# Making the token operand sums of a two-layer gated MLP on VectorE instead of Pool

## The reference

```
attention, per batch b (8) and head h (8), S = 576 tokens, D = 64:
    kv  = k^T v                      # 64 x 64
    o   = q kv                       # no softmax
    x   = o / sqrt(mean(o*o) + 1e-6) * g_norm
x: 4608 tokens x 512
layer 1:  x = (sigmoid(x Wg) * (x Wv)) Wo        # 512 -> 1536 -> 512
layer 2:  g = x Wg2;  x = (g * sigmoid(g) * (x Wv2)) Wo2
```

## Time and profile before

| what | value |
|---|---|
| time, median of 3 runs | 1890.42 us (1886.0 to 1890.89) |
| the profiled execution's own time | 1887.9 us |
| its span | 1886.1 us |
| mean granted TensorE clock | 0.98 of 2.4 GHz |
| busy share, TensorE / VectorE / ScalarE / Pool | 94% / 69% / 47% / 25% |
| Pool's four sums, 12 each | 22.8 + 24.5 + 26.6 + 22.8 us |
| VectorE's split of a token operand, 60 + 24 | mean 1209 and 1055 ns |

### The profile page before, as it was taken

One profiled execution on the slowest core, in us unless ns is written; L12 is line 12 of the kernel. 1 busy time (PEld: TensorE's weight loads), 2 busy tenths in 40 slices (PEclk: granted clock), 3 DMA queues, 4 the chain that ended last, 5 costly groups with the idle time before them and its releaser, 6 DMA issues.

```text
span 1886.1 us, 30995 instructions
## 1 busy us (share of the span) xinstructions
PE 1774.4 (94%) x11184; PEld 1729.8 (92%) x11184; DVE 1297.9 (69%) x1993; ACT 892.7 (47%) x1676; POOL 462.8 (25%) x374
## 2 busy tenths in 40 slices
PE   6898999999999999999987999998999998999997
PEld 5787898899999999999987999998999998999997
DVE  3566767777765678666678777777767778766665
ACT  3555655555444445444354444444444444544444
POOL 5623323213211124111135011113211124111111
PEclk9999999999999999999999899999999999999998
DMA  8677587556655666665555544545665565555452
GB/s 204 211 220 235 185 252 237 190 183 202 229 187 208 209 223 226 210 212 185 185 179 190 185 161 174 185 167 197 214 208 186 184 220 195 172 182 182 183 183 75
DMA packets 201561, 368.52 MB, mean 195 GB/s; under 512 B 49856, under 2 KB 161472, under 8 KB 201408
## 3 DMA queue, kind: packets, MB, share of 16 engines
q1 hardware_dynamic: 201408, 366.53, 58.0%
HBM read 234.36 MB, written 130.55 MB: 193 GB/s over the span
## 4 chain that ended last, share of the span: by engine, by line
PE 71%; DVE 10%; issue 7%; DMA 4%; POOL 3%; SPq 2%; ACT 2%; POOLq 0%; DVEq 0%; ACTq 0%
PE ps L687 68%; DVE arena L1075 2%; DVE xo L984 2%; DVE hop L1036 2%; DVE arena L1088 1%; PE ps L595 1%; PE ps L628 1%; POOL rrms L1210 1%; DVE arena L1103 1%; DMA wops<-in_moe_w_gate_dram 1%; DMA x<-wops 1%; DMA wops<-in_v_dram 1%; DVE wa L979 1%; DMA wops<-in_q_dram 1%; PE ps L580 1%
## 5 line engine op out<-in xcount | busy, mean ns | idle before, releaser
L687 PE MATMUL ps<-xo,wa 128*128 128x384 f32 x6048 | 1087.0, 337 | 16.0 <-ACT arena L845 8.7
L687 PEld LDWEIGHTS ps<-xo,wa 128*128 128x128 f32 x6048 | 1051.1, 189 | 22.6 <-ACT arena L845 11.1
L687 PE MATMUL ps<-hop,wb 128*128 128x384 f32 x3024 | 562.7, 345 | 53.7 <-DVE arena L1088 23.4
L1075 DVE TENSOR_TENSOR arena<-ps,arena 128x384 f32<-128x384 f32 x648 | 351.2, 552 | 366.6 <-PE ps L687 287.0
L687 PEld LDWEIGHTS ps<-hop,wb 128*128 128x128 f32 x3024 | 541.6, 194 | 65.9 <-DVE arena L1088 25.3
L845 ACT ACTIVATE arena<-ps 128x384 f32<-128x384 f32 x648 | 317.4, 491 | 595.1 <-PE ps L687 583.2
L1292 POOL TENSOR_TENSOR arena<-arena 128x384 f32<-128x384 f32 x144 | 144.7, 1028 | 762.6 <-DVE arena L1075 762.6
L1036 DVE TENSOR_TENSOR hop<-arena,hop 128x384 fp32r<-128x384 f32 (+1 forms) x396 | 304.8, 792 | 37.2 <-ACT hop L827 31.2
L827 ACT ACTIVATE hop<-arena 128x384 fp32r<-128x384 f32 (+1 forms) x396 | 233.4, 608 | 66.7 <-DVE arena L1103 38.7
L866 ACT ACTIVATE arena<-arena 128x384 f32<-128x384 f32 x216 | 112.6, 521 | 118.2 <-DVE arena L1075 118.2
L1103 DVE TENSOR_TENSOR arena<-arena 128x384 f32<-128x384 f32 x216 | 143.3, 664 | 13.5
(11 more groups left out here) (61 smaller groups left out, 972.7 us busy)
## 6 DMA issues: line engine op xcount, KB each, us to landing
xo<-x_operands SPq DMA_DIRECT2D x168, 768.0 KB, 6.3
x_operands<-xo SPq DMA_DIRECT2D x84, 768.0 KB, 4.6
x<-arena SPq DMA_DIRECT2D x120, 384.0 KB, 3.3
arena<-x SPq DMA_DIRECT2D x96, 384.0 KB, 4.4
xraw<-x SPq DMA_DIRECT2D x22, 768.0 KB, 6.7
out_dram<-wops SPq DMA_DIRECT2D x48, 192.0 KB, 2.1
wops<-in_k_dram SPq DMA_DIRECT2D x22, 288.0 KB, 4.5
wops<-in_v_dram SPq DMA_DIRECT2D x22, 288.0 KB, 5.3
```

The source lines that it names most:

```text
L687: mm = pe.matmul(dst, lhsT, rhs, start=(pr in (1, 5, 2) and c == 0 and i == 0), stop=(c == 1 and i == 2), skip_group_check=(pr in (6, 7, 4 ...
L1075: nc.vector.tensor_tensor(dst, acc, buf, ALU.add).then_inc(summed, 1)
```

## The change

Pool no longer makes the token sums. VectorE makes all four with the same operands: `x_s1_s3` (s1 and, after it, s3), `x_s2` and `x_s4`. In a preparing stage s1 and s3 stand in window 2 where split 5 stood; after total(22,1) come split 5 and s2; split 6 stays. s4 and split 7 go to the head of window 0 of the next stage, ahead of splits 4 and 3. X_ORDER has 6 before 7. ScalarE's halves: split 5 at slot 7, split 6 at slot 9 as before, split 7 at slot 13. The DRAM store of operand 7 is issued in the next stage. For block 0 VectorE does s1, s3, split 5, s2, split 6 ahead of the loop, and s4, split 7 in stage 0.

```diff
-X_ORDER = (1, 2, 5, 7, 6, 4, 3)
+X_ORDER = (1, 2, 5, 6, 7, 4, 3)
...
-            for pr in X_ORDER[2:5]:
+            for pr in X_ORDER[2:4]:
                 store_xo(0, pr)
...
                 if first_pass(qq):
-                    for pr in X_ORDER[5:]:
+                    for pr in X_ORDER[4:]:
                         store_xo(qq, pr)
...
-                if prepares:
-                    store_xo(nxt, X_ORDER[4])
...
                             if is_late(u - 1):
                                 unit_xT(u - 1)
-                            if w == 2 and prepares:
-                                split_x(nxt, 5)
                         if s == 7:
                             copy(7, 0)
                             if w < 2:
...
                             if w == 2 and prepares:
-                                split_x(nxt, 7)
+                                split_x(nxt, 5)
...
                         if s == 12 and w == 2 and p == 0:
                             copy_c21(1)
-                        if s == 13 and is_late(u):
-                            unit_xT(u)
+                        if s == 13:
+                            if w == 2 and prepares:
+                                split_x(nxt, 7)
+                            if is_late(u):
+                                unit_xT(u)
...
+            a11, a12, a21, a22 = xraw[:, 0, 0:2], xraw[:, 0, 2:4], xraw[:, 1, 0:2], xraw[:, 1, 2:4]
+
+            def x_s1_s3(qq):
+                if qq == 0:
+                    for filled in x_filled:
+                        dve.wait_ge(filled, 48)
+                else:
+                    for loaded in xraw_loaded:
+                        dve.wait_ge(loaded, 16 * prep(qq))
+                nc.vector.tensor_tensor(xs, a21, a22, ALU.add).then_inc(xs_made, 1)
+                dve.wait_ge(xs_made, 4 * prep(qq) + 1)
+                nc.vector.tensor_tensor(a21, a11, a21, ALU.subtract).then_inc(xs_made, 1)
+
+            def x_s2(qq):
+                dve.wait_ge(x_lo, n_x(qq, 1))
+                dve.wait_ge(xs_made, 4 * prep(qq) + 2)
+                nc.vector.tensor_tensor(a11, xs, a11, ALU.subtract).then_inc(xs_made, 1)
+
+            def x_s4(qq):
+                dve.wait_ge(x_lo, n_x(qq, 5))
+                dve.wait_ge(xs_made, 4 * prep(qq) + 3)
+                nc.vector.tensor_tensor(xs, a12, a11, ALU.subtract).then_inc(xs_made, 1)
+
...
-            for pr in X_ORDER[2:5]:
-                split_x(0, pr)
+            x_s1_s3(0)
+            split_x(0, 5)
+            x_s2(0)
+            split_x(0, 6)
...
                         if w == 0 and first_pass(qq):
+                            x_s4(qq)
+                            split_x(qq, 7)
                             split_x(qq, 4)
                             split_x(qq, 3)
...
                         total(11, 0)
                         hop_split(3, None)
                         if prepares:
-                            split_x(nxt, 5)
+                            x_s1_s3(nxt)
                         total(22, 0)
                         if is_late(u):
                             unit_scale(u)
                         total(11, 1)
                         total(22, 1)
                         if prepares:
-                            split_x(nxt, 7)
+                            split_x(nxt, 5)
+                            x_s2(nxt)
...
-            x_s1(0)
-            x_s3(0)
-            x_s2(0)
-            x_s4(0)
...
-                if prepares:
-                    x_s1(nxt)
-                u = late_unit(qq, 2)
-                if is_late(u):
-                    rsqrt(u)
-                if prepares:
-                    x_s3(nxt)
-                    x_s2(nxt)
-                    x_s4(nxt)
-                if is_late(u + 1):
-                    rsqrt(u + 1)
+                for u in range(late_unit(qq, 2), late_unit(qq, 2) + 2):
+                    if is_late(u):
+                        rsqrt(u)
```

More of the change, by code:

```diff
@@ L1220, in differences @@
                 nc.gpsimd.tensor_tensor(st[:, 6], st[:, 3], st[:, 5], ALU.subtract).then_inc(t_made, 1)
[L1222 to L1245, removed]
             for t in range(STEPS):
@@ L1259, in _ @@
                 nxt = qq + 1
-                prepares = first_pass(nxt)
                 first_unit = 6 * (qq // NB + 1) if blk == NB - 1 and nxt < QN else None
```

## The result

| | before | after |
|---|---|---|
| time, median | 1890.66 us (1886.0 to 1891.87, 4 runs) | 1856.95 us (1854.75 to 1858.37, 4 runs) |
| the profiled execution, its span | 1887.9, 1886.1 us | 1854.75, 1853.0 us |

The account below looks back on a forecast made before the run. TensorE bounds the kernel, held by VectorE's chain that Pool's sums stretch by 4.3 us. Terms -18.5 - 1.4 - 2.9 - 3.1 - 7.3 = -33.2 gave 1854.7 us profiled, median 1857; range 1840 to 1876.

Parts of the forecast that it names:

- Rival 2: VectorE's chain before window 2: lengthening not from Pool, nothing gained there and tails paid, about 1915 us; chance 0.05.
- entry: Entry to window 2, stages 19 to 22: 0.55 us of waiting left of 4.20, and the clock stays up.
- tail: End of window 2, every prepared stage: waits of 0.7 before product 3 and 0.9 before the next stage, together 1.6 us.
- rival 1: Tail of window 2 is longer, 3.2 us, since ScalarE stands twice before a late VectorE sum: 1875 us; chance 0.15.
- rival 4: Tail of window 2 hides, bank waits only 0.3 us: 14 us better, 1843 us; chance 0.12.
- rival 3: Gain given back to the second-slowest chain, entry waits near 2.5 us, clock still falling: about 1871 to 1885; chance 0.11.
- The 1.68 us wait for hidden operand 7 stays: Stages 0 to 2: this wait remains because Pool's rsqrt starts in front of it; these stages -3.1 us in all.
- the store of operand 7: DMA queue at the next stage's head: it moves behind the next unit's loads, is read one pass later, costs nothing.
- stage 3: Wait of 2.88 us shrinks to 0.45, tail costs 1.4: -2.9 us.
- Stage 17: Pool's weight differences take the place of its sums in window 2, where the wait was 2.54 us: -0.8 in all.
- Stage 18: -3.0 us from additions L1292 no longer late, and -3.5 from the shrunken wait of 7.36 us.
- the term of -3.5: Stage 18: wait of 7.36 us shrinks to 2.8, with half of the clock's loss left standing.

Follow-up runs that it names:

- Experiment 1: The kernel before, with each of Pool's four token sums covering one column of 384 (results wrong): 1826.49 us, ratio 0.968.
- Experiment 3: The changed kernel's order of splits, stores and X_ORDER, with the four sums made by Pool at their places of before: 1901.81 us, ratio 1.0079.
- experiment 4: The changed kernel with three idle Pool instructions (96x768, two SBUF inputs) added in each of stages 17 to 22: 1882.01 us, ratio 0.9981.
- Experiment 6: The changed kernel, with the next attention unit's loads in window 2 issued ahead of the store of operand 5 in the DMA queue: 1852.4 us, ratio 0.9807.
- Experiment 10: The changed kernel with unit loads earlier in the DMA queue in windows 0, 1 and 2, copies ahead of split 6, s3 behind total(22,0): 1833.22 us.
- experiment 2: The changed kernel, with each of VectorE's four token sums covering one column of 384 (results wrong): 1838.76 us, ratio 0.9746.

## Why the prediction was right

*What bounds the kernel, and why.* This is right, and shown: experiments 1, 3 and 4 remove, keep and restore the wait with the reading Pool work alone. Rival 2 (the lengthening isn't Pool's) fell with the changed kernel's 0.55 us silu and with experiment 4. The rule of the Trainium skill, "SBUF — State Buffer", section "Who interferes with whom", says as well that a GpSimd instruction which only writes doesn't contend; the 0.55, 0.56 and 0.95 us beside eight memsets agree.

*Entry and tail.* The entry was predicted at 0.55 us, and 0.7 was found. The tail was predicted at 0.7 + 0.9 = 1.6. The rows show 0.48 and 0.50 of idle time (0.65 and 0.67 with the pipelined end), and taking both waits away brings the stage from 45.99 to 44.43 us, so it is 1.56. Rivals 1 (3.2 us) and 4 (0.3 us) are out, and rival 3 as well: no entry wait of 2.5 us is left.

*The rest of the sum is right partly by luck.* That the profiled execution came out at 1854.75 us, where 1854.7 was forecast, is chance: the parts outside stages 19 to 22 and stage 4 were off by up to 2.3 us each way and cancelled. These steps were wrong:

- "The 1.68 us wait for hidden operand 7 stays, because Pool's rsqrt starts in front of it": wrong in its cause. In the kernel before, the two splits of 5.08 us at 141.34 had two Pool instructions beside them:
```profile
140.60 2.96 POOL L1210 TENSOR_TENSOR rrms<-msq,mhalf 96x12 f32<-96x12 f32 x1 [7.50 <-DVE msq L999]
141.34 2.59 DVE L1036 TENSOR_TENSOR hop<-arena,hop 128x768 fp32r<-128x768 f32 x1
...
143.53 2.08 POOL L1235 TENSOR_TENSOR xraw<-xraw 128x768 f32<-128x768 f32 x1
```
  After, the rsqrt is still there and the splits are short:
```profile
142.31 2.94 POOL L1238 TENSOR_TENSOR rrms<-msq,mhalf 96x12 f32<-96x12 f32 x1 [8.74 <-DVE msq L998]
...
143.04 1.84 DVE L1061 TENSOR_TENSOR hop<-arena,hop 128x768 fp32r<-128x768 f32 x2
```
  In the whole kernel after, 15 splits of 128x768 ran beside an rsqrt and no other Pool instruction, and took 0.94 to 0.97 us each. In the kernel before three of them also touched s3's record, one in each of stages 0 to 2, and took 2.58. Experiment 1 shows the same pair at 1.84 us beside the rsqrt (2.94 us at 141.88), in the old order, with s3 of one column behind it. So the lengthening goes with s3's size and not with the rsqrt. How is open: the first split ends at 143.93, 0.4 us after s3's recorded start, so it was late before the record shows s3 at work (a Pool span in the records is rough). Window 2 of stage 0 fell from 26.12 to 22.39 us.
- The queue of DMAs. I priced the store of operand 7 at nothing and overlooked that of operand 5: it now waits for the later split 5 and holds the next attention unit's loads, issued at 151.62 where they were issued at 150.23, while TensorE wants v 1.4 us earlier (at 156.18, not 157.57). The wait that this leaves, in the timeline after:
```profile
151.22 0.35 SPq L408 DMA_DIRECT2D x_operands<-xo  x1
151.62 0.43 SPq L342 DMA_DIRECT2D wops<-in_k_dram  x1
...
158.07 0.92 PE L578 MATMUL ps<-wops 96*64 96x64 f32 x24 [1.89 <-DMA wops<-in_v_dram]
```
  There are two more like it, 1.99 (229.57) and 1.94 us (298.64), in stages 2 and 3, and none at these places before. A fourth, of 1.97 at 183.34, is not new: in the kernel before it is 2.57 (182.29). Experiment 6 shows that the three new ones come from the queue's order; with them gone stage 3 is 3.3 us shorter than before, where 2.9 was predicted and 0.6 measured. Experiment 10 gives 14 us more, but it goes further than undoing what the change did to the queue: it also takes away waits that the kernel before had.
- Stage 17. The wait of 2.54 us for a split of a hidden operand is gone, but the wait for a product behind the first step has grown from 1.36 to 2.95 us (972.10), and product 3 waits 1.32 us. Before, it was
```profile
977.45 7.58 PE L687 MATMUL ps<-hop,wb 128*128 128x384 f32 x42 [1.36 <-DVE arena L1103]
```
  Stage 17 is 1.0 us longer, not 0.8 shorter.
- Stage 18. It gained 9.35 us where 6.5 was predicted. The wait fell from 7.36 to 2.65, close to the 2.8 predicted, but the term of -3.5 does not follow from its own numbers: 7.36 - 2.8 is 4.6 already, half of the clock's loss is 1.3 more, and a tail of 1.6 goes the other way, together -4.3. Measured are -4.71 for this wait and +0.51 for window 2 behind it, thus -4.2. The other -5.15 lie in windows 0 and 1, where -3.0 was predicted for the additions L1292.
- The order of the work. The sum prices the later places of splits and stores at nothing except in the tail. Experiment 3 (15 us slower than before) and the pair of experiments 1 and 2 (12 us) show that it costs more, in stages 0 to 3 above all. Experiment 1 shows what the end of the contention is worth by itself in stages 0 to 3, 17.4 us; the change kept 5.9 of it, and the sum said 6.0. That is right, but with a gain and a cost that are both larger than the sum had them.

## What to carry to other kernels

A Pool instruction costs what VectorE can't do while it runs, not its own busy time: look for VectorE instructions with two SBUF inputs that take a multiple of their usual time beside one, while PSUM readers keep theirs, and move the work there if VectorE is the engine that the bottleneck waits for. When a stall goes, the next wait is often in the queues: read for each DMA queue which store is held by a later producer, and what loads stand behind it. Waits on one chain must be taken away together: here the first alone gave 0.1 us a stage, the last alone 0.8, and both 1.56.

## What the runs showed of the hardware that was not expected

A long Pool instruction need not hold VectorE: the 96x12 rsqrt ran for 2.94 us with two splits inside it that took their usual 1.84 together, though both kinds read two SBUF inputs, while the 128x768 sums of 2 us held VectorE's instructions. The rule that the prediction quotes does not tell these two apart. With a full sum queued behind the rsqrt, the split of 141.34 should have ended at 142.3 and was still running when the sum's record starts (143.53), so the record of Pool alone doesn't tell which instruction holds. Writes from Pool stretched nothing on VectorE: eight memsets in 6.30 us. And VectorE makes such a sum in 0.95 us where Pool took 1.85 even with little beside it (1.84 us at 1122.16 in the kernel of experiment 3).
